# Attention and two MLPs on one core: the sums for the last score tile are read from DRAM, and POOL's order of work in a slot is changed

## The reference

```python
def _attn_ref(q, k, v, s):                   # 4 batches, 8 heads, 576 positions, 64 wide
    scores = (1/sqrt(64)) * q @ k^T
    cum = np.cumsum(np.maximum(s, 0.0), axis=-1)
    bias = -(cum[:, :, :, None] - cum[:, :, None, :])
    scores = np.where(causal, -1e9, scores + np.minimum(bias, 0.0))
    attn = exp(scores - max); attn = attn / (sum + 1e-9)
    return attn @ v
x = attention output as (2304, 512)
x = (h - tanh(h)) @ w_out,          h = x @ w_in            # 512 -> 2048 -> 512
x = layernorm(h * softmax(h)) * g_ln @ w2_out,  h = x @ w2_in   # 512 -> 1024 -> 512
```

## Time and profile before

| what | value |
|---|---|
| median of 3 runs | 823.18 us (821.99 to 823.32) |
| profiled execution, its own time | 824.0 us |
| its span, first to last instruction | 822.2 us |
| PE busy | 800.8 us (97%) |
| DVE, ACT, POOL busy | 471.5, 396.2, 280.4 us |
| mean granted clock of TensorE | 0.994 |

### The profile page before, as it was taken

The page is one execution under the profiler, slowest core; times in us unless marked ns, Lnnn a source line. Parts: engine busy times, 40 slices in busy tenths (PEclk is TensorE's granted clock), DMA queues, the critical chain, the costliest instruction groups (busy, mean ns, idle before and its releaser), DMA issues. The chain is left out here.

```text
span 822.2 us, 14626 instructions
## 1 busy us (share of the span) xinstructions
PE 800.8 (97%) x4498; PEld 670.5 (82%) x4498; DVE 471.5 (57%) x1101; ACT 396.2 (48%) x935; POOL 280.4 (34%) x322
## 2 busy tenths in 40 slices
PE   6999999998999999999999999999999899999998
PEld 5888888887888889988888888887887788888886
DVE  5889888888754342432233222446667666666662
ACT  5999899887544332322232222324434344343332
POOL 4687787778100000000000000035554644444400
PEclk9999999999999999999999999999999999999999
DMA  6656555544342300000000000002000000000001
GB/s 174 165 149 160 140 140 154 146 113 144 101 141 82 102 1 1 1 1 1 0 1 0 0 0 0 1 0 91 13 0 1 27 26 27 26 13 26 13 26 51
DMA packets 77722, 46.39 MB, mean 56 GB/s; under 512 B 59824, under 2 KB 68144, under 8 KB 77680
## 3 DMA queue, kind: packets, MB, share of 16 engines
q1 hardware_dynamic: 75232, 45.19, 19.2%
q10 hardware_dynamic: 2448, 0.66, 0.4%
HBM read 40.97 MB, written 4.87 MB: 56 GB/s over the span
## 5 line engine op out<-in xcount | busy, mean ns | idle before, releaser
L1456 PE MATMUL psum<-x_hi,w1i 128*128 128x512 f32 (+1 forms) x640 | 182.0, 369 | 0.1
L1469 PE MATMUL psum<-gate_hi,w1o 128*128 128x512 f32 (+1 forms) x640 | 146.2, 370 | 1.9 <-DVE gate_lo L1152 1.9
L1456 PEld LDWEIGHTS psum<-x_hi,w1i 128*128 128x128 f32 x640 | 115.6, 188 | 20.8 <-DVE w1i L1109 0.5
L1469 PEld LDWEIGHTS psum<-gate_hi,w1o 128*128 128x128 f32 x640 | 112.3, 188 | 23.7 <-DVE gate_lo L1152 2.7
L1152 DVE TENSOR_TENSOR gate_lo<-gate,gate_hi 128x512 fp32r<-128x512 f32 (+1 forms) x80 | 55.4, 692 | 123.0 <-ACT gate_hi L859 122.9
L1456 PE MATMUL psum<-x_lo,w1i 128*128 128x512 f32 (+1 forms) x320 | 117.7, 368 | 0.0
L712 POOL TENSOR_TENSOR w2t<-stage 128x512 f32<-128x512 f32 x2 | 5.7, 2858 | 325.7 <-PE psum L1469 325.7
L859 ACT ACTIVATE gate_hi<-gate 128x512 fp32r<-128x512 f32 (+1 forms) x80 | 47.2, 590 | 132.1 <-PE psum L1469 123.2
L1140 DVE TENSOR_TENSOR gate<-psum,gate 128x512 f32<-128x512 f32 (+1 forms) x80 | 51.0, 638 | 94.7 <-ACT gate L846 93.1
L846 ACT ACTIVATE gate<-psum 128x512 f32<-128x512 f32 (+1 forms) x80 | 44.4, 555 | 117.0 <-PE psum L1456 86.8
L884 ACT ACTIVATE probs<-probs,neg_max 128x128 f32<-128x128 f32 (+2 forms) x144 | 83.6, 587 | 10.3 <-DVE neg_max L1185 10.0
(11 more groups left out here) (154 smaller groups left out, 1419.3 us busy)
## 6 DMA issues: line engine op xcount, KB each, us to landing
cum_bc<-cum_dram SPq DMA_DIRECT2D x16, 576.0 KB, 4.6
rden_T<-rden_dram SPq DMA_DIRECT2D x32, 144.0 KB, 3.0
out_x<-out_sb SPq DMA_DIRECT2D x18, 256.0 KB, 2.0
stage<-in_q SPq DMA_DIRECT2D x32, 128.0 KB, 2.4
v_raw<-in_v SPq DMA_DIRECT2D x32, 128.0 KB, 3.6
stage<-in_moe_w_in SPq DMA_DIRECT2D x16, 256.0 KB, 3.0
stage<-in_moe_w_out SPq DMA_DIRECT2D x16, 256.0 KB, 3.5
stage<-in_k SPq DMA_DIRECT2D x28, 128.0 KB, 2.3
```

The source lines that it names most:

```text
L1456: mm = pe.matmul(h_ps[j % 4][:, 0:wide(c)], wp[j][:, kt, :], xp[:, kt, 0:wide(c)], start=(n == 0), stop=(n == 3 * KT - 1))
L1469: mm = pe.matmul(y_ps[m][:, 0:wide(c)], wp[j][:, m * P:(m + 1) * P], gp[j % 2][:, 0:wide(c)], start=(j == 0 and wp is w1o_hi and gp is gat ...
```

## The change

The two copies of POOL are gone. In their place SP issues, in slot s between cum_bc of pair s+1 and v of pair s, two transfers that read one row of cum_dram each to 64 partitions of cum_tail. They wait for the biased tiles of pair s-1, the last readers of cum_tail. DVE's last tile waits for these two transfers. POOL's list becomes: split_qk(0..2), first_x in two slots, the high part of v, scale_x, the low part of v. Several of POOL's waits on its own earlier instructions are left out.

```diff
@@ semaphores
+        cum_tail_in = sem("cum_tail_in")
-        cum_copied = sem("cum_copied")
@@ SP, slot
                 if sl.runs(0):
                     pair, half, par = sl.pair(0)
                     wait(sp, v_split, 2 * (pair - 1))
+                    wait(sp, biased, TILES * pair)
                     met(sp)
+
+                    for h in range(2):
+                        sp.dma_start(cum_tail[h * TAIL:(h + 1) * TAIL, :],
+                                     cum_dram[bass.ds(2 * pair + h, 1), :].to_broadcast([TAIL, S])).then_inc(cum_tail_in, 16)
                     load_rows(sp, v_raw[par], v_pairs, pair, v_in[par])
                     load_tail(sp, v_raw[par], v_pairs, pair, v_in[par])
@@ POOL, slot
-                def sums():
-
-                    if sl.runs(0):
-                        pair, half, par = sl.pair(0)
-                        pool.wait_ge(cum_in[par], 16 * (half + 1))
-                        wait(pool, biased, TILES * pair)
-                        wait(pool, v_split, 2 * pair)
-                        met(pool)
-                        pool.tensor_copy(cum_tail[0:TAIL, :], cum_bc[par][0:TAIL, 0, :]).then_inc(cum_copied, 1)
-                        pool.wait_ge(cum_copied, 2 * pair + 1)
-                        met(pool)
-                        pool.tensor_copy(cum_tail[TAIL:P, :], cum_bc[par][TAIL:P, 1, :]).then_inc(cum_copied, 1)
-
                 def split_qk(n):
...
                         pool.wait_ge(qk_copied, 3 * pair + n + 1)
-                        if n == 0:
-                            pool.wait_ge(cum_copied, 2 * (pair - 1) + 2)
-                        else:
-                            pool.wait_ge(qk_lo, 3 * pair + n)
...
                         pool.wait_ge(rden_in[par], 32 * (half + 1))
-                        if sl.runs(1):
-                            pool.wait_ge(qk_lo, 3 * sl.pair(1)[0] + 3)
-                        elif sl.runs(0):
-                            pool.wait_ge(cum_copied, 2 * sl.pair(0)[0] + 2)
-                        else:
-                            pool.wait_ge(x_done, pair)
                         pool.wait_ge(x_added, 2 * pair + 2)
...
-                def split_v():
+                def v_hi():
                     if sl.runs(0):
                         pair, half, par = sl.pair(0)
-                        raw = v_raw[par].rearrange("p t (h d) -> p t h d", h=2)
                         pool.wait_ge(v_in[par], 48 * (half + 1))
-                        pool.wait_ge(cum_copied, 2 * pair + 2)
-                        if sl.runs(1) and not (sl.fixed and sl.s <= 0):
-                            pool.wait_ge(qk_lo, 3 * sl.pair(1)[0] + 3)
-                        wait(pool, x_done, pair - 1)
                         wait(pool, attended, 2 * (pair - 1))
                         met(pool)
-                        pool.tensor_copy(high(v_parts[par]), raw).then_inc(v_split, 1)
+                        pool.tensor_copy(high(v_parts[par]), v_raw[par].rearrange("p t (h d) -> p t h d", h=2)).then_inc(v_split, 1)
+
+                def v_lo():
+                    if sl.runs(0):
+                        pair, half, par = sl.pair(0)
                         pool.wait_ge(v_split, 2 * pair + 1)
                         met(pool)
-                        pool.tensor_tensor(low(v_parts[par]), raw, high(v_parts[par]).bitcast(F32),
-                                           ALU.subtract).then_inc(v_split, 1)
+                        pool.tensor_tensor(low(v_parts[par]), v_raw[par].rearrange("p t (h d) -> p t h d", h=2),
+                                           high(v_parts[par]).bitcast(F32), ALU.subtract).then_inc(v_split, 1)
...
-                sums()
                 split_qk(0)
                 split_qk(1)
                 split_qk(2)
                 if sl.fixed and sl.s == PAIRS - 1:
                     first_x(0, 1, 2)
-                    pool.wait_ge(x_lo_done, 3)
                 if sl.fixed and sl.s == PAIRS:
                     first_x(3)
-                    pool.wait_ge(x_lo_done, 4)
+                v_hi()
                 scale_x()
-                split_v()
+                v_lo()
@@ DVE, bias
                         if h is None:
-                            dve.wait_ge(cum_copied, 2 * (pair + 1))
+                            dve.wait_ge(cum_tail_in, 32 * (pair + 1))
```

More of the change, by code:

```diff
@@ L654, in scale_x @@
                         pool.tensor_tensor(dst, x_sum[:, :], rden_T[par][:, :], ALU.mult).then_inc(x_done, 1)
-                def split_v():
+                def v_hi():
                     if sl.runs(0):
                         pair, half, par = sl.pair(0)
-                        raw = v_raw[par].rearrange("p t (h d) -> p t h d", h=2)
                         pool.wait_ge(v_in[par], 48 * (half + 1))
-                        pool.wait_ge(cum_copied, 2 * pair + 2)
-                        if sl.runs(1) and not (sl.fixed and sl.s <= 0):
-                            pool.wait_ge(qk_lo, 3 * sl.pair(1)[0] + 3)
-                        wait(pool, x_done, pair - 1)
                         wait(pool, attended, 2 * (pair - 1))
                         met(pool)
-                        pool.tensor_copy(high(v_parts[par]), raw).then_inc(v_split, 1)
+                        pool.tensor_copy(high(v_parts[par]), v_raw[par].rearrange("p t (h d) -> p t h d", h=2)).then_inc(v_split, 1)
+                def v_lo():
+                    if sl.runs(0):
+                        pair, half, par = sl.pair(0)
                         pool.wait_ge(v_split, 2 * pair + 1)
                         met(pool)
-                        pool.tensor_tensor(low(v_parts[par]), raw, high(v_parts[par]).bitcast(F32),
-                                           ALU.subtract).then_inc(v_split, 1)
+                        pool.tensor_tensor(low(v_parts[par]), v_raw[par].rearrange("p t (h d) -> p t h d", h=2),
+                                           high(v_parts[par]).bitcast(F32), ALU.subtract).then_inc(v_split, 1)
                 def first_x(*tiles):
                     for kt in tiles:
-                        pool.wait_ge(cum_copied, 2 * PAIRS)
-                        wait(pool, x_lo_done, kt)
                         pool.tensor_copy(x_hi[:, kt, :], xT[:, kt, 0:CH]).then_inc(x_hi_done, 1)
```

## The result

The changed kernel takes **828.9 us** (median of 5 runs, 826.96 to 830.82) against 823.18 us (5 runs, 821.99 to 823.48). The ratio is 1.0075, with a 95% interval of 1.0055 to 1.0095: slower by some 5.7 us. The profiled execution has 830.82 us, the slowest of the five, and a span of 828.8.

The account below looks back on a forecast made before the run. POOL's 12.3 us list was taken to bound slots 7 to 14. The attention ends 4.1 us later, start-up's 0.9 included: 823.18 + 4.1, rounded up to 827.4 us; own range 824.5 to 830.5, 8 in 10 range 822.2 to 831.5.

Parts of the forecast that it names:

- The bound before: Attention slots 7 to 14: POOL's 12.3 us list bounds, PE stands 0.55 us behind; 5.4 us lost over slots 6 to 15.
- SP's list becomes the longest: Loop slots: two added issues make SP's list 11.5 + 1.55 = 13.05 us, longer than POOL's list was.
- When the delay reaches PE: Attention loop: SP is the bound from slot 8 on; slots 8 to 13 take 13 us each instead of 12.28.
- The lag limits for v and for cum_tail: Loop slots: SP may lag PE by 5.0 us before v's lateness delays PE, and by 4.8 for cum_tail.
- The start-up term: Slot 0: DVE's last tile waits for cum_tail until 15.4, a delay of 0.9 us, with 0 and 1.4 as ends.
- The attention's end: Slots 14 to 16: POOL's list, then DVE's x_add, lets PE go on at 206.2 instead of 202.06, 4.1 us later.
- S + 8.05: Earliest start of PE's next slot, through v, scale_x and x_add; S is the start of cum_bc in a slot.
- the clock falls: Rival, SP-bound slots: PE's idle lowers its clock, costing 1 us in every second of eight slots, 831 us; chance 0.15.
- POOL's missing waits: POOL's slots: leaving out waits on its own finished work shortens gaps of 0.17 to 0.35 us a little, counted at nothing.

Follow-up runs that it names:

- e2: As e1, but cum_tail is loaded for pair 0 only and used for every pair, so the output is wrong: 819.11 us, ratio 0.9932.
- e4: Changed kernel with cum_tail again made by POOL's two copies and SP's list as before; POOL's new order and left-out waits stay: 818.07 us, ratio 0.9921.
- e6: As e4, but in POOL's old order, so only the waits on its own finished work are gone: 817.27 us, ratio 0.9924.
- e3: As e1, but from pair 1 on the two transfers bring 16 of 576 columns, so the output is wrong: 825.16 us, ratio 1.0014.
- e8: As e4, but SP brings the same bytes in three more issues per slot, for cum_bc and v's rows: 828.87 us, ratio 1.0052.
- e9: Kernel before with the two transfers replacing POOL's copies; POOL keeps its old order and its waits on its own work: 827.67 us, ratio 1.0052.
- e10: As e1, but SP issues the two reads of cum_tail ahead of cum_bc of the next pair: 824.62 us, ratio 1.0014.
- e1: Changed kernel with cum_tail of pair 0 loaded in slot -1, right behind the first cum_bc: 825.78 us, ratio 1.0028.
- e5: As e1, but cum_tail comes by one transfer to 128 partitions instead of two to 64: 871.33 us, ratio 1.0563.

## Why the prediction was right, and where its terms were off

The forecast was 827.4 us, and 828.9 was measured. The mechanism is the one that was forecast; that the number came so close is partly luck. In the profiled execution, 1.9 us above the median, errors of 3.0 us at the start and 1.4 at the end stood against 2.4 in the length of SP's list and 1.4 that came back in the MLPs.

**The bound before, and PE 0.55 us behind it: right.** Taking POOL's list below PE's gives slots of 11.78 us to the end (e2, e4, e6) and 4 to 6 us, where 5.4 was read off.

**SP's list becomes the longest: right, and shown twice over.** 13.05 us were forecast, 12.8 measured. The pair costs 1.15 to 1.19 instead of 1.31, the row of cum_dram being issued in 0.48 us where line 535's takes 0.57. The list has 17 issues a slot and had 15, not the twelve that the prediction speaks of; its sum does not use that count. e3 shows that it is issue time and not bytes, e8 that such a list alone has the effect, e9 that POOL's half doesn't matter beside it. cum_bc of slot 14 was put at 185.2 and went out at 186.81. The loop began 3.0 us later than forecast (57.04 against 54.0), and its first two slots took 27.8 us (57.04 to 84.84) against 27.1; the other eight took 102.0 against 104.4.

**When the delay reaches PE: the slot right, the first wait the second of the two named.** The lag limits for v and for cum_tail were worked out as 5.0 and 4.8 and called the same. (The 5.0 is for a period of 13.05; at PE's own 11.74 the same sum gives 3.7, and the count for slot 8 rightly used that pace.) In slot 7 SP was 5.03 us behind PE and cost nothing, in slot 8 it was 6.20 behind and PE waited. It was cum_tail, with PE's wait at the first scores and not inside the slot; e10 brings out the other at nearly the same cost. Slot 8 was forecast to start late; it ended late.

**The start-up term failed in size.** The step "I take 15.4, a delay of 0.9 us, with 0 and 1.4 as ends" is wrong. The last tile of slot 0 started at 17.62:

```profile
17.62 0.76 DVE L1162 CUSTOM_DVE_ANT_0 probs<-psum,cum_tail 128x576 f32<-128x576 f32 x1 [2.78 <-DMA cum_tail<-cum_dram]
```

3.1 us late. PE behind it came back at the lower clock and kept it to about 26 us, 5 us of its work; before, it did so for 3. That is the other 0.8. The step took 3.0 to 4.6 us to landing from medians over the whole run. The second of these two issues landed 6.1 us after it went out, at 17.41, the longest of all 32 (3.0 at least, 4.6 at the median). The 576 KB of cum_bc and loads of q went out just ahead of it; that they are the reason is argued. e1 gives 3 to 4 us of it back.

**The attention's end: 4.1 forecast, 8.0 measured; the path that was priced is not the one that ended last.** The step that led to 206.2 followed POOL's list from slot 14 to the scale_x of slot 15. That list came out as forecast: scale_x began at 204.67 and ended at 206.11, 19.3 us after slot 14's cum_bc, where 20.1 was put. But PE went on at 210.06. What DVE's x_add waited for at this place, before and after:

```profile
201.25 0.75 DVE L1208 TENSOR_TENSOR x_sum<-psum,x_low 64x576 f32<-64x576 f32 x1 [1.54 <-POOL xT L654]
```
```profile
209.26 0.75 DVE L1185 TENSOR_TENSOR x_sum<-psum,x_low 64x576 f32<-64x576 f32 x1 [1.07 <-ACT x_low L902]
```

Before, POOL was last. Now POOL had been done for 3.2 us, and the chain through PE's own slot 15 was last: PE goes on 14.4 us after the start of slot 15 at 195.67. The prediction's own limit for that start, S + 8.05, gives 207.6 by this chain, so 1.4 us were missing from the forecast. The other 2.4 of the 3.9 are 1.6 by which slot 14's cum_bc was later (186.81), where the start-up ends up, and 0.8 by which slot 15 began later than S + 8.05.

**The clock in the loop: a rival that took place in part.** After the wait of 2.05 us that ended at 118.24 PE ran at the lower of its two levels, 1.2 GHz, for about three us, and again after one of 1.50 that ended at 182.50. After 2.22 us, ended at 157.31, it did not. One window behind each of the three, in order of time (PEclk is the third value from the end):

```profile
119.00:120.00 1.00, 1.00 (x11) 0.78 (x10) 0.25 (x1) 0.94 (x3) 1.00 (x1) 0.50 0.33 75
...
158.30:159.30 1.00, 1.00 (x12) 0.94 (x11) 0.53 (x4) 0.85 (x3) 1.00 (x1) 1.00 0.00 1
...
183.50:184.50 1.00, 1.00 (x9) 1.00 (x8) 0.10 (x1) 0.74 (x2) 1.00 (x2) 0.50 0.03 8
```

So the rival "the clock falls" took place in two of the seven slots in this execution. Slots 8 to 14 take 13.06 us each where SP's list is 12.8, 1.8 us in all. Most of that is not the clock: PE began slot 8 with SP 6.20 us behind it and slot 14 with SP 4.31 behind, so that PE's six slots from 8 to 13 had to take 1.9 us longer than SP's. In slot 9 DVE still waited 0.30 us for cum_tail, so that the lower clock cost nothing beyond SP's bound there. In slot 14 it did: the slot took 13.17 us without a wait where PE's pace is 11.8, and DVE's last tile began at 194.49, 0.9 us after cum_tail had landed (193.57), where in slots 8, 11 and 13 it began 0.27 after. By this the clock cost some 0.6 us in all, an estimate; no run kept the waits and not the clock. The last 1.4 us between 8.0 and the span's 6.6 come back in the MLPs, where the change does nothing; what gave them is open. The five runs spread over 4 us.

**POOL's missing waits: the step "I count them at nothing because POOL has slack by then" was right for the sum and wrong as reading.** Within this change the slack made it true. But the gaps of 0.17 to 0.65 us that stood in the earlier trace rows are worth the whole gain by themselves: in the kernel before, where POOL is the bound, leaving out the waits gives 0.9924 (e6), and leaving out the waits and the copies with no transfer in the loop in their place gives 0.9932 (e2). What the copies alone are worth no run shows.

## What to carry to other kernels

Before moving work to a queue that only issues transfers, add up its own list for one turn (issue times and the gaps between them) and compare it with the pace of the engines; a queue without a wait in its view sets the pace of whatever depends on it, whatever the busy shares say. If an in-order engine is the bound, look first for waits on its own last instruction that no data requires: here leaving them out gave some 6 us, with no transfer added (e6, 817.27 us, is faster than both kernels), while the whole change lost 5.7. A delay on such a queue has no single place; taking one wait away (e10) brings up the next.

## What was unexpected of the hardware

- On POOL, an instruction without a wait starts 0.04 to 0.06 us before the end shown for the one ahead (111.60 + 0.71 against 112.27). A wait on the one ahead costs 0.16 to 0.18 us, and 0.65 us where computed addresses stand behind the wait (scale_x in the loop, with 0.22 us of register work in the trace), against 0.17 in the written-out slots.
- The same broadcast of 288 KB lands 3.0 to 6.1 us after issue as two transfers to 64 partitions each, and as one with a dimension of 2 outermost too late in 14 slots, with 0.13 of the DMA engines busy (e5, 46 us more than e1). The issue behind it on SP could take 4.38 us instead of 0.66.
- PE's waits of 1.50 and 2.05 us were followed by the lower granted clock, one of 2.22 us was not.
- An issue on SP takes as long for 16 columns as for 576: 0.48 us at the median in both.
